# Two feed-forward layers in float32 halves: from two token tilings with one matrix in the 7-product form to 768-token blocks with both matrices in it

## The reference, cut to what matters

```python
def _moe_ref(x, w_in, w_out):          # w_in 512 x 2048, w_out 2048 x 512
    h = x @ w_in
    g = h * (1.0 / (1.0 + np.exp(-h)))
    return (g @ w_out).astype(np.float32)
# the second layer is the same with exp(-1.702 * h)
```

## Time and profile before

| | us |
|---|---|
| median of 3 runs (lowest, highest) | 916.94 (915.94, 918.65) |
| the profiled execution | 916.11 |
| its span, first to last instruction | 914.3 |
| busy in it: TensorE matmul, VectorE, ScalarE, GpSimd | 882.0, 422.1, 363.0, 307.4 |
| mean granted TensorE clock | 0.989 of full |

### The profile page before, as it was taken

The page is one execution under the profiler, slowest core; times in us unless marked ns, Lnnn a source line. Parts: engine busy times, 40 slices in busy tenths (PEclk is TensorE's granted clock), DMA queues, the critical chain, the costliest instruction groups (busy, mean ns, idle before and its releaser), DMA issues.

```text
span 914.3 us, 16560 instructions
## 1 busy us (share of the span) xinstructions
PE 882.0 (96%) x6555; PEld 790.3 (86%) x6555; DVE 422.1 (46%) x662; ACT 363.0 (40%) x754; POOL 307.4 (34%) x251
## 2 busy tenths in 40 slices
PE   7999969799999999999999899999999999999998
PEld 4787869799999999999999798899999999999997
DVE  7888957455533333323333454654333343333332
ACT  4676666344342243224333345434422332242221
POOL 5556669855160014004022357451600150040000
PEclk9999989899999999999999999999999999999999
DMA  5666565466554445554566223865564446545541
GB/s 156 169 168 190 151 198 192 162 258 225 213 193 174 161 162 178 194 191 163 207 214 247 93 85 125 314 235 202 190 240 164 162 165 227 197 183 185 184 162 47
DMA packets 33212, 167.48 MB, mean 183 GB/s; under 512 B 2977, under 2 KB 13569, under 8 KB 24961
## 3 DMA queue, kind: packets, MB, share of 16 engines
q1 hardware_dynamic: 33152, 166.65, 52.0%
HBM read 132.56 MB, written 34.08 MB: 182 GB/s over the span
## 4 chain that ended last, share of the span: by engine, by line
PE 77%; POOL 4%; DVE 2%; ACT 2%; issue 1%; ACTq 0%; POOLq 0%; DVEq 0%
PE hid L247 38%; PE yp L307 20%; PE yp L303 19%; POOL xs L459 1%; DVE win L411 1%; POOL win_raw L490 1%; ACT win L341 1%; POOL wout L498 1%; POOL win_raw L489 0%; POOL win_raw L492 0%; POOL win_raw L494 0%; ACT win L338 0%; ACT xs L328 0%; ACT gs L352 0%; DVE x L426 0%
## 5 line engine op out<-in xcount | busy, mean ns | idle before, releaser
L247 PEld LDWEIGHTS hid<-xs,win 128*128 128x128 f32 x3072 | 383.7, 194 | 27.3 <-issue 13.1
L247 PE MATMUL hid<-xs,win 128*128 128x256 f32 x3072 | 387.4, 285 | 20.0 <-POOL xs L459 8.1
L303 PE MATMUL yp<-gs,wout 128*128 128x512 f32 (+1 forms) x960 | 204.5, 369 | 0.0
L307 PE MATMUL yp<-wout,gs 128*128 128x512 f32 x864 | 203.2, 390 | 0.0
L303 PEld LDWEIGHTS yp<-gs,wout 128*128 128x128 f32 x960 | 165.8, 189 | 28.2
L307 PEld LDWEIGHTS yp<-wout,gs 128*128 128x128 f32 x864 | 159.7, 188 | 31.5
L419 DVE TENSOR_TENSOR gs<-g,gs 128x1024 fp32r<-128x1024 f32 (+1 forms) x80 | 102.9, 1286 | 130.2 <-ACT gs L352 130.2
L459 POOL TENSOR_TENSOR xs<-x,xs 128x512 fp32r<-128x512 f32 x28 | 43.1, 1555 | 317.7 <-ACT xs L328 317.7
L387 ACT ACTIVATE p<-hid 128x256 f32<-128x256 f32 x64 | 24.6, 384 | 219.6 <-PE hid L247 219.6
L351 ACT ACTIVATE g<-hid 128x256 f32<-128x256 f32 x96 | 36.8, 383 | 181.3 <-PE hid L247 180.8
L436 DVE TENSOR_TENSOR hv<-p,hid 128x256 f32<-128x256 f32 x64 | 26.9, 421 | 165.6 <-PE hid L247 165.5
(11 more groups left out here) (71 smaller groups left out, 690.0 us busy)
## 6 DMA issues: line engine op xcount, KB each, us to landing
win<-win_split SPq DMA_DIRECT2D x48, 1792.0 KB, 7.3
win_split<-win SPq DMA_DIRECT2D x16, 1792.0 KB, 6.6
win_raw<-in_w_in SPq DMA_DIRECT2D x32, 512.0 KB, 4.7
qk<-in_qkT SPq DMA_DIRECT2D x16, 576.0 KB, 5.0
wout_raw<-in_w_out SPq DMA_DIRECT2D x16, 512.0 KB, 4.6
vn<-in_v SPq DMA_DIRECT2D x16, 288.0 KB
out<-x SPq DMA_DIRECT2D x18, 256.0 KB, 8.2
vwin<-in_v SPq DMA_DIRECT2D x16, 245.0 KB
```

The costliest lines, as they stand in the source:

```text
L247: last = eng.matmul(to, lhsT=win[:, s.k % 2, w, weights(s, a), cc * P:(cc + 1) * P], rhs=xs[:, part, q, cc * 256:(cc + 1) * 256], start=st ...
L303: last = eng.matmul(yp[:, m, 0:s.tokens], lhsT=wout[:, s.p, w, f, m * P:(m + 1) * P], rhs=chunk[:, 0:s.tokens], start=start, stop=stop)
L307: last = eng.matmul(yp[:, m, :], lhsT=chunk[:, m * P:(m + 1) * P], rhs=wout[:, s.p, w, f, :], start=start, stop=stop)
```

## The change

The feed-forward part is rewritten. A layer is 3 blocks of 768 tokens, in halves of 384. A block has two phases:

- Phase one is 8 pairs. In each, 7 products of 6 matmuls with 384 columns give the four hidden tiles, which are gated and kept as float32 in `G` for all 8 pairs.
- Phase two computes the output matrix in the 7-product form too: 7 products, each over all 8 pairs, 48 matmuls of 384 columns. For each product after the first, the needed operand is taken from `G` and split into `gr` (one buffer), two pairs at a time, as soon as TensorE has read the two pairs that were there.

Weights are no longer kept split. Each block reads its float32 operands again from device memory, in 30 batches of 3 or 4 tiles of 128 x 256, and splits every batch in `wh` (3 slots). The sums of quarters are made once per matrix by GpSimd and kept in device memory: those of the first matrix during attention, the other three during phase one of blocks 0, 1 and 2. The features are in device memory between the stages (`xb`): attention stores each unit's result there, each block loads its 768 tokens into `xt`, and each block stores its results. VectorE forms the differences of x and all rests of x; it also takes the rests of batches 0 to 19, and GpSimd those of 20 to 29. The layout of the returned array is changed back outside the timed program.

The core of the diff (the new lists of the engines; helpers of one line are left out):

```diff
+FIRST = ((A11, B11, 0, True), (S2, T2, 1, True), (S1, T1, 2, True), (S3, T3, 3, True),
+         (A12, B21, 0, False), (S4, B22, 2, False), (A22, T4, 3, False))
+SECOND = ((A11, G11, True), (S1, G11, True), (A12, G21, False), (S4, G22, False),
+          (S3, G12, True), (S2, GT2, True), (A22, G21, False))
...
+    BLOCKS, PAIRS, HALF = 3, 8, 384
+    BATCHES = 30
+    RAWS, SLOTS = 4, 3
...
         @block.tensor
+            def first(n, p):
...
+                    for cc in range(2):
+                        for j, (part, rest) in enumerate(((0, 0), (0, 1), (1, 0))):
+                            last = eng.matmul(
+                                hid[:, at, 0:HALF], lhsT=wh[:, w % SLOTS, part, a % 4, cc * P:(cc + 1) * P],
+                                rhs=xs[:, rest, q, cc, :], ...
+            def second(n, i):
...
+                for p in range(PAIRS):
+                    w = BATCHES * n + 16 + 2 * i + p // 4
+                    if p % 4 == 0:
+                        split(eng, w)
+                    if i == 0:
+                        eng.wait_ge(self.b11_lo, PAIRS * n + p + 1)
+                    elif p % 2 == 0:
+                        eng.wait_ge(self.g_lo, 24 * n + 4 * (i - 1) + p // 2 + 1)
+                    for m in range(2):
+                        for j, (part, rest) in enumerate(((0, 0), (0, 1), (1, 0))):
+                            last = eng.matmul(
+                                yp[:, at + m, 0:HALF], lhsT=wh[:, w % SLOTS, part, p % 4, m * P:(m + 1) * P],
+                                rhs=gr[:, p, rest, :], ...
+                    if p % 2:
+                        last.then_inc(pair, 1)
...
         @block.scalar
+            def first(n, p):
+                s, w, scale = PAIRS * n + p, BATCHES * n + 2 * p, self.GATE[layer_of(n)]
+                eng.wait_ge(product, 7 * s + 1)
...
+                eng.activation(p1[:], hid[:, 0, 0:HALF], ACT.Copy).then_inc(self.p1_copy, 1)
+                if p:
+                    gate_rest(s - 1, scale)
+                round_weights(w + SLOTS)
...
+                eng.wait_ge(product, 7 * s + 5)
+                eng.activation(G[:, p, G11, :], hid[:, 0, 0:HALF], ACT.Silu, scale=scale)
+                eng.activation(gr[:, p, 0, :], hid[:, 0, 0:HALF], ACT.Silu, scale=scale).then_inc(self.gate, 1)
+                round_weights(w + 1 + SLOTS)
...
+            def second(n, i):
+                w = BATCHES * n + 16 + 2 * i
+                if i == 0:
+                    gate_rest(PAIRS * n + 7, self.GATE[layer_of(n)])
+                for a in range(4):
+                    if i < 6:
+                        round_gates(n, i + 1, a)
+                    if a == 1:
+                        round_weights(w + SLOTS)
+                    if a == 2:
+                        round_x(n + 1, i)
+                if i < 5:
+                    copy_out(n, i)
+                round_weights(w + 1 + SLOTS)
...
         @block.vector
+            def rest_weights(w):
...
+                eng.tensor_tensor(wh[:, w % SLOTS, 1, 0:e, :], raw(w), wh[:, w % SLOTS, 0, 0:e, :].bitcast(F32),
+                                  ALU.subtract).then_inc(w_lo_v, 1)
+            def prepare_x(n, i):
...
+                rest_x(n, i)
+                for q in {B11: (T1, T2), T1: (T3,), B21: (T4,)}.get(i, ()):
+                    sum_x(n, q)
...
+            def rest_gates(n, i, a):
+                eng.wait_ge(self.g_hi, 24 * n + 4 * (i - 1) + a + 1)
+                eng.tensor_tensor(gr[:, 2 * a:2 * a + 2, 1, :], G[:, 2 * a:2 * a + 2, SECOND[i][1], :],
+                                  gr[:, 2 * a:2 * a + 2, 0, :].bitcast(F32), ALU.subtract).then_inc(self.g_lo, 1)
...
+            def second(n, i):
+                w = BATCHES * n + 16 + 2 * i
+                for a in range(4):
+                    if i < 6:
+                        rest_gates(n, i + 1, a)
+                    if a == 1:
+                        rest_weights(w + SLOTS)
+                    if a == 2:
+                        prepare_x(n + 1, i)
+                if i == 6:
+                    results(n)
+                rest_weights(w + 1 + SLOTS)
...
         @block.gpsimd
+            for n in range(N):
+                for p in range(PAIRS):
+                    if n < 3:
+                        sum_pair(8 * n + p)
+                    if p:
+                        sum_gates(PAIRS * n + p - 1)
+                sum_gates(PAIRS * n + 7)
+                for a in range(4):
+                    sum_t2(n, a)
+                for k in range(20, BATCHES):
+                    rest_weights(BATCHES * n + k)
+                    if 21 <= k < 25:
+                        sum_t4(n, k - 21)
...
         @block.sync
+            def batch(w):
...
+                        store_first(p + 2)
+                    if n < 3:
+                        if k % 2:
+                            store_pair(8 * n + p)
+                        elif p:
+                            load_pair(8 * n + p + 1)
...
+                load_batch(w + RAWS)
...
 def build(nc, qkT, v, w_in, w_out, out, heads):
-        x = keep("x", [P, NC, T])
+            xo = sb("xo", [P, 2, S])
...
+                def store_x(u):
+                    eng.wait_ge(x_done, 1 + u.n + 1)
+                    at = (2 * (u.half % 2) + u.odd) * T + (u.half // 2) * S
+                    to = ffn.xb[0].rearrange("p c n -> p (c n)")
+                    eng.dma_start(to[:, bass.ds(at, S)], xo[:, u.odd, :]).then_inc(x_out[u.odd], DMA_INC)
...
+                for n in range(UNITS - 2, UNITS):
+                    store_x(Unit(n // 2, n % 2))
+                for done in x_out:
+                    eng.wait_ge(done, 1 + DMA_INC * UNITS // 2)
```

More of the change, by code:

```diff
@@ L116, in block_fills @@
-    def block_fills(self, block):
-        before = 0
-        for n in range(block):
-            before += 2 if n % Step.BLOCKS == 0 else 7
-        order = (FILLS_PLAIN, FILLS_AFTER_PLAIN, FILLS, FILLS, FILLS)[block % Step.BLOCKS]
-        return {q: before + i + 1 for i, q in enumerate(order)}
-    def vacated(self, block, q):
-        for n in range(block - 1, -1, -1):
-            end = self.steps[n * Step.PAIRS + Step.PAIRS - 1]
-            done = DONE_PLAIN if end.plain else DONE
-            if q in done:
-                return end.h(done[q])
-        return 0
@@ L214, in banks, with layer_of @@
[L214 to L233 removed]
+        def layer_of(n):
+            return n // self.BLOCKS
@@ L529, in store @@
-            def store(s):
-                for m in range(banks(s)):
-                    who, done = (0, self.y_act) if m < banks(s) // 2 else (1, self.y_dve)
-                    eng.wait_ge(done, y_copies(s.block, who) + m % (banks(s) // 2) + 1)
-                    row = s.first + m * P
-                    dst, _ = y_view(s, m)
-                    to = self.out[row:row + P, :]
-                    if s.plain:
-                        to = to.rearrange("p (a n) -> p a n", a=2)
-                    eng.dma_start(to, dst).then_inc(self.stored, DMA_INC)
@@ L570, in build @@
+            store_first(0)
+            store_first(1)
+            for w in range(LAST + 1):
+                batch(w)
+            eng.wait_ge(self.y_sum, 5 * N)
+            store(N - 1, 2)
+            eng.wait_ge(self.y_out, stored(N))
 def build(nc, qkT, v, w_in, w_out, out, heads):
```

816 lines of the change are left out of this document (407 added, 409 removed).

## The result

The changed kernel takes 999.77 us, median of 4 runs (994.21 to 1003.15), against 917.79 (915.94 to 918.65) for the kernel before in the same runs: ratio 1.089, 95% interval 1.0835 to 1.0945. It is slower, as forecast, but by 82 us where 36 were forecast, and the time lies outside the range of 912 to 988. The profiled execution took 1001.02 us with a span of 999.2.

The account below looks back on a forecast made before the run. TensorE, busy 96%, was taken to bound the kernel. Block 0's phase one ending at 200.9, five more 292.0, five phases two 384.0, the last 64.0, early blocks 3, attention 3, tail 4: span 951, so 953 us; range 912 to 988.

Parts of the forecast that it names:

- TensorE's pace: Feed-forward matmuls: 4032 of 384 columns at 173.9 ns, 701 us against 763, a gain of 62.
- 17.4 of turns and 1.0 of clock: Phase two: turns plus idle make 75.8 us, 17.4 over TensorE's 58.4; lost clock adds 1.0, giving 76.8 a block.
- the order of the lists: Phase two: in-order lists and single `gr` leave turns idle, stopping TensorE in products 1 and 3; 75.8 us instead of 72.6.
- the sum of turns: Phase two: VectorE's 30.1 and GpSimd's 38.1 us alternate at SBUF, 68.2 together, at least 72.6 with both ends.
- The last block: Its phase two prepares no x: turns of 58.9 us, 63.3 with both ends, taken as 64.
- It fits; I add 3 us: Phase one: engine work and turns fit in a pair's 7.30 us; 3 us added for all three early blocks together.
- rival C: Phase one of blocks 1 and 2: DMA at 250 GB/s makes a pair 9.4 us, 34 us more, 987; chance 0.12.
- The first pair: Feed-forward start: first pair ends 24 us after entry, at 149.8; store and load cycle 14 to 15 us, slots covering the rest.
- The 3 us were for bandwidth: Attention: added DMA traffic brings its share near 0.9, costing 0 to 8 us, taken as 3.
- GpSimd's two additions a unit: Attention: two additions of 256, 1.5 us a unit, hidden in 2.53 us of idle; if not, 24 us.
- Rival A: Phase two: turns don't bind, so it takes TensorE's 58.4 us and the kernel 855, faster than before; chance 0.11.
- Rival B: Phase two: turns at their minimum, 72.6 us a block without clock loss, kernel 929; chance 0.2 with its neighbourhood.

Follow-up runs that it names:

- The experiment on the order: Changed kernel with the next block's x prepared at the end of each product instead of between its gates: 1003.38 us, ratio 1.0957.
- T2 early: Changed kernel with GpSimd forming the T2 sums in phase one, pair by pair, instead of in phase two: 968.13 us, ratio 1.0561.
- weights on VectorE: Changed kernel with VectorE taking the rests of all 30 weight batches and GpSimd none: 948.97 us, ratio 1.0352.
- three later kernels: Changed kernel with all mends together, x at product ends (902.51 us) or between gates (896.84), and the latter with SyncE's seam transfers reordered (894.91).
- the PSUM kernel: Changed kernel with the rests of gates subtracting an idle PSUM tile, so the rests are wrong numbers: 905.07 us, ratio 0.9883.
- the old-order kernel: Changed kernel with attention, T2, weight-rest and pair-spreading mends together, x still prepared before the last pair of gates: 896.84 us, ratio 0.9764.

## Why the prediction was right and wrong

Its span of 951 against 999.2, term by term (measured minus predicted):

| term | predicted | measured | difference |
|---|---|---|---|
| attention's last matmul (120.9 + 3) | 123.9 | 141.2 | +17.3 |
| from there to the end of the first pair | 28.9 | 29.3 | +0.4 |
| the rest of phases one (51.1 + 292 + 3) | 346.1 | 372.6 | +26.5 |
| five phases two | 384.0 | 383.8 | -0.2 |
| the last phase two | 64 | 68.3 | +4.3 |
| tail | 4 | 3.9 | -0.1 |

The end of the first pair is taken at 170.5: ScalarE's next rounding waits for it and starts at 170.64.

*TensorE's pace: right.* 173.9 ns by interpolation, 174.1 measured. The 62 us were real.

*Phase two: right in size and in the turns, not in the part of the order.* The idle time before the last two pairs of product 1 was 7.00 us against 7.7 worked out from alternating turns, and product 3's 4.94 against 6.6. The account of block 0's phase two is: 13.5 us idle plus 4.9 more busy (63.4 against 58.5) make 76.9. Most of the 4.9 is TensorE's clock, which was granted at 0.66 on average in the 6 us after the first stop and at 0.69 from 267 to 275, about 4 us lost together. The prediction had it as 17.4 of turns and 1.0 of clock, so the total agrees and the split does not; that the five phases agree to 0.2 us is luck. (The prediction's 1.7 and 3.3 us of clock, for the stops before the change, are too high as well: those groups took 4.37 us where 24 such matmuls take 3.04, and 7.98 where 42 take 5.20, so 1.3 and 2.8 were lost.) The working named the order of the lists as the reason for 75.8 instead of 72.6. The experiment on the order contradicts that: another order did not reach 73, nor gain anything. That half of the step was only argued, and what puts the phase above the sum of turns is open. What is shown is that turns are the cause (949 against 1962 ns, 76.9 against 60.2 us), and that fewer turns shorten the phase.

*The last block: mis-sized by 4.3.* TensorE's granted clock was 1.00 there, so it isn't the clock. 58.9 us of turns with both ends gave 63.3. It is still turns: with the rests of gates reading PSUM this phase took 58.4. What the sum leaves out is when they fall. Up to 974 TensorE stops before every two pairs, twelve times in the phase and 6.4 us in all, because a rest of gates is ready only every 2.6 to 3.0 us, one for each instruction of GpSimd (T4 sums of 2.56 us and batches of 3.12 in turn), where TensorE takes 2.1 for two pairs. The last 120 matmuls then run without a stop:

```profile
948.82 2.35 PE L245 MATMUL yp<-gr,wh 128*128 128x384 f32 x12 [0.65 <-DVE gr L414]
...
974.31 21.04 PE L245 MATMUL yp<-gr,wh 128*128 128x384 f32 x120 [0.78 <-DVE gr L414]
```

So the turns that stand in the first five products bound those, and the free time after them comes too late. T2 early and weights on VectorE took the phase to 63.8 and 63.6, which is above their sums too.

*Phase one: the step that failed.* "It fits; I add 3 us" was worked out from engine times and turns; the same phase's DMA load stood in rival C and was left out of the sum. Blocks 1 and 2 cost 29 us there, against 34 worked out for C at 250 GB/s (the stretch moved 262); 20 of the 29 are the transfers'. The figure that failed stands under "The first pair": a store and a load of a pair at "about 5 us each", which "give a cycle of two pairs in 14 to 15 us", with "four raw slots cover the rest". The store of 896 KB took 7.8 us to landing in the median and up to 11.5, and SyncE's list has the wait for it once in every pair, so two buffers of sums do not overlap. The raw loads came 8.3 to 13.2 us apart (17.8 us for two pairs at the least), and the batches, which stand behind them in the list, were issued after their buffers had become free. Four slots cover 14.6 us only if the batches are issued when a slot is free. Rival C had named SyncE's waits for landings in its favour, and the prediction gave it too little weight. Also, the additions and the transfers don't just add: with either gone 8.4 or 20.3 us come back, with both 28.2.

*Attention: the step that failed.* The 3 us were for bandwidth, and 17.3 were measured (12 to 17 over the kernels with attention unedited, which differ by up to 5.7 us for which no cause was looked for). A large part of the cost was the position of the store in SyncE's list: behind a wait and behind other loads, so that two buffers of output were not enough, and VectorE, in order, held everything behind its wait. Moving two steps, with the bytes unchanged, brought its end to 125.8, close to the forecast's 123.9; three later kernels with the same list had 127.8, 131.7 and 131.6. So the place of these issues costs 4 to 15 us, and what is left above 123.9 in the slower ones (waits for q and k) is open. The prediction had counted the bytes and not the place. GpSimd's two additions a unit are hidden for the most part, as forecast: they are in the kernel that ended at 125.8, 4.9 us after the kernel before, where 24 us were the price if not.

*The first pair and the seam: right within about 1 us.* The feed-forward part is entered at 147.2, and the pair ends 23.3 us later, against 24 worked out; TensorE's longest stop in it (3.32 us) ends with a rest of x by VectorE, which fits the prediction's account. That the seam's length hangs partly on the order of transfers at the seam was not foreseen.

*The chances.* Rival A was given 0.11 and would need the interface free; the PSUM kernel shows what it would have brought: 905, not 855, because in that kernel attention ended 13.5 us later than forecast, phases one of blocks 1 and 2 took 22 us more than forecast and the five phases two 12 (304.3 against 292). Its evidence was also put too strongly: the prices of a turn were taken from the same six turns that "end to 0.01 us where alternation puts them", and only the repeated 1.08 and VectorE's 0.55 for half the elements test them to 0.01; GpSimd's 1.16 for half of 2.27 is 0.02 off. Rival B, with 929, had the same omission. The range's upper end was set by C alone, added to nothing; C and late stores together went beyond it.

## What to carry to other kernels

When an engine's work is moved to VectorE and GpSimd, add up their turns, VectorE's with both sources in SBUF and GpSimd's, as if it were one engine's work. Here that sum was a lower bound: with about 73, 66, 61 and 55 us (both ends included) the phases with x to prepare took 76 to 79, 69 to 74, 67 to 74 and 61 to 66, where TensorE needs 58.5. Look also at when the turns fall, since those in the first products can't use the free time of the last. Taking work out of the sum helped each time (a source in PSUM, the engine whose turn is shorter, a phase where TensorE has slack); the one other order tried did not.

Read the list of the queue that issues transfers as closely as an engine's: for each store, what stands before it and who waits for its landing, and for each wait for a landing, which issues stand behind it. A transfer that adds little to the mean bandwidth still costs a stall where a large one is issued just ahead of the small one that is wanted next.

## What the runs showed that was not expected

- A tensor-scalar of VectorE on 3 columns seems to wait for GpSimd too, and without taking a turn in between: in the old-order kernel it starts at 121.49 and ends at 123.60, when three GpSimd instructions that began from 121.48 on are done (the same line takes 0.17 us at its shortest). This is one instance; its cause was not tested.

```profile
121.48 0.73 POOL L865 TENSOR_TENSOR vavg<-vpair 72x256 f32<-72x256 f32 x1
121.49 2.11 DVE L981 TENSOR_SCALAR nga<-mxa 96x3 f32<-96x3 f32 x1
122.17 0.72 POOL L880 TENSOR_TENSOR G<-G  x1
122.85 0.73 POOL L881 TENSOR_TENSOR G<-G  x1
```

- The landing of a transfer depended more on what was issued before it than on its size: a 288 KB store behind 2.5 MB kept VectorE waiting 9.23 us, and a batch of 512 KB, 4.5 us in the median, kept ScalarE waiting 8.49 behind x and a store of sums.
- The order that was expected to be better was the worse one: with the turns reduced, preparing x at the end of a product made three phases two 1.8 to 2.9 us longer than preparing it between the gates, and one 0.8 shorter.
